# One level of Strassen's scheme for the x w_a and x w_b products of two gated layers, in tiles of 768 tokens

## The reference, cut to what matters

```python
def _attn_ref(q, k, v, g_norm):            # q, k, v: 4 batches, 8 heads, 576 tokens, 64
    kv = np.einsum('bhsd,bhse->bhde', k, v)
    out = np.einsum('bhsd,bhde->bhse', q, kv)
    rms = np.sqrt(np.mean(out * out, axis=-1, keepdims=True) + 1e-06)
    return (out / rms * g_norm).astype(np.float32)

def _moe_ref(x, w_a, w_b, w_out):          # x: 2304 x 512, w_a, w_b: 512 x 1536, w_out: 1536 x 512
    return (((x @ w_a) * (x @ w_b)) @ w_out).astype(np.float32)

def _moe2_ref(x, w_gate, w_val, w_out):
    gate = 1.0 / (1.0 + np.exp(-(x @ w_gate)))
    return ((gate * (x @ w_val)) @ w_out).astype(np.float32)
```

## Time and profile before

| | us |
|---|---|
| runs shown: median (lowest to highest, 3 runs) | 1001.93 (998.65 to 1002.4) |
| profiled execution: span from first to last instruction | 998.2 |
| median less span | 3.7 |
| attention, up to the first matmul of a layer | 93.3 |
| the two layers, to the last matmul | 901.5 |
| TensorE busy | 978.8 (98%) |
| DVE busy / ACT busy / POOL busy | 508.2 / 444.2 / 16.7 |

### The profile page before, as it was taken

One profiled execution on the slowest core, in us unless ns is written; L12 is line 12 of the kernel. 1 busy time (PEld: TensorE's weight loads), 2 busy tenths in 40 slices (PEclk: granted clock), 3 DMA queues, 4 the chain that ended last, 5 costly groups with the idle time before them and its releaser, 6 DMA issues.

```text
span 998.2 us, 14895 instructions
## 1 busy us (share of the span) xinstructions
PE 978.8 (98%) x5744; PEld 945.2 (95%) x5744; DVE 508.2 (51%) x742; ACT 444.2 (45%) x755; POOL 16.7 (2%) x84
## 2 busy tenths in 40 slices
PE   7799999999999999999999999999999999999998
PEld 7688999999999999999999999999999999999997
DVE  1357545545545545545545545545545545545543
ACT  2368434434434434434434434434434435434433
POOL 1112000000000000000000000000000000000000
PEclk8899999999999999999999999999999999999999
DMA  9995200000000000000543000000000000000000
GB/s 230 241 245 158 78 1 0 0 0 0 0 0 0 0 0 0 0 0 1 150 126 105 1 1 32 0 0 32 0 0 32 0 0 31 0 0 27 6 1 32
DMA packets 41132, 38.15 MB, mean 38 GB/s; under 512 B 1936, under 2 KB 35728, under 8 KB 41104
## 3 DMA queue, kind: packets, MB, share of 16 engines
q1 hardware_dynamic: 41104, 37.76, 14.5%
HBM read 33.03 MB, written 4.72 MB: 38 GB/s over the span
## 4 chain that ended last, share of the span: by engine, by line
PE 93%; DMA 2%; SPq 2%; ACT 1%; DVE 0%; issue 0%; POOL 0%; POOLq 0%
PE bank L372 60%; PE bank L419 15%; PE bank L421 15%; DMA qkv_even<-in_v_dram 2%; SPq L215 2%; PE bank L330 1%; PE bank L344 1%; PE bank L355 1%; ACT x L466 1%; PE bank L318 0%; ACT squares L452 0%; DVE normed L563 0%; ACT qT L442 0%; SPq L239 0%; DVE kv L538 0%
## 5 line engine op out<-in xcount | busy, mean ns | idle before, releaser
L372 PE MATMUL bank<-x_hi,ab_hi 128*128 128x384 f32 x1152 | 385.7, 335 | 0.0
L372 PE MATMUL bank<-x_hi,ab_lo 128*128 128x384 f32 x1152 | 385.7, 335 | 0.0
L372 PE MATMUL bank<-x_lo,ab_hi 128*128 128x384 f32 x1152 | 385.3, 334 | 0.0
L585 DVE TENSOR_TENSOR wo_lo<-w_raw,wo_hi 128x512 fp32r<-128x512 f32 x144 | 99.5, 691 | 236.1 <-ACT wo_hi L485 236.1
L372 PEld LDWEIGHTS bank<-x_hi,ab_hi 128*128 128x128 f32 x1152 | 216.3, 188 | 2.9
L372 PEld LDWEIGHTS bank<-x_lo,ab_hi 128*128 128x128 f32 x1152 | 216.3, 188 | 2.8
L372 PEld LDWEIGHTS bank<-x_hi,ab_lo 128*128 128x128 f32 x1152 | 216.2, 188 | 0.0
L572 DVE TENSOR_TENSOR ab_lo<-w_raw,ab_hi 128x1024 fp32r<-128x1024 f32 x144 | 176.3, 1225 | 53.2 <-ACT ab_hi L471 52.1
L488 ACT ACTIVATE h_hi<-qkv_even 128x384 fp32r<-128x384 f32 x144 | 75.8, 526 | 248.3 <-DVE qkv_even L589 248.3
L482 ACT ACTIVATE qkv_even<-bank 128x384 f32<-128x384 f32 x144 | 70.9, 492 | 254.4 <-PE bank L372 254.2
L471 ACT ACTIVATE ab_hi<-w_raw 128x1024 fp32r<-128x1024 f32 x144 | 150.4, 1044 | 0.0
(11 more groups left out here) (49 smaller groups left out, 533.0 us busy)
## 6 DMA issues: line engine op xcount, KB each, us to landing
w_raw<-in_moe_w_out_dram SPq DMA_DIRECT2D x24, 256.0 KB, 4.4
out_dram<-qkv_even SPq DMA_DIRECT2D x18, 256.0 KB, 2.0
w_raw<-in_moe_w_a_dram SPq DMA_DIRECT2D x12, 256.0 KB, 5.3
w_raw<-in_moe_w_b_dram SPq DMA_DIRECT2D x12, 256.0 KB, 5.6
w_raw<-in_moe_w_gate_dram SPq DMA_DIRECT2D x12, 256.0 KB, 3.0
w_raw<-in_moe_w_val_dram SPq DMA_DIRECT2D x12, 256.0 KB, 3.4
w_raw<-in_q_dram SPq DMA_DIRECT2D x2, 1152.0 KB, 17.1
qkv_even<-in_k_dram SPq DMA_DIRECT2D x4, 288.0 KB, 5.3
```

The lines of the kernel that those rows point to most:

```text
L372: last = pe.matmul(acc[:, 0:TILE], w[:, m % 2, at], xx[:, c, :], start=(c == 0 and n_pass == 0), stop=(c == KC - 1 and n_pass == 2))
L585: dve.tensor_tensor(wo_lo[:, m % 2, :], w_raw[:, m, 2 * HALF:3 * HALF], wo_hi[:, m % 2, :].bitcast(F32), ALU.subtract).then_inc(wo_lo_read ...
```

## The change

The hidden products of both layers are computed by Winograd's form of Strassen's scheme. The unit is 512 features by 256 hidden features (one of w_a or w_b, so 12 units in a tile) by 768 tokens. Cut in two along each side it is eight block products; the scheme makes seven, each of 6 matmuls of 384 columns (2 chunks of features times 3 passes). It needs four sums of weight blocks per unit and four sums of token blocks per tile (both on POOL, into `s_raw` and `t_raw`), and seven sums or copies of the block products per unit: in `bank[0]` to `bank[3]` three products are added to what four others left there. All seven weight blocks (14 x 128 columns per unit) and all seven token blocks (5376 columns per tile) are split into hi and lo.

The tile grows from 384 to 768 tokens, 3 per layer. TensorE runs `project` of an earlier hidden chunk in pairs of matmuls between the products of a unit. A tile has 24 project steps (12 chunks, 2 halves of 384 tokens): 10 beside units 2 to 11, and 14 behind them. The first half's accumulators are drained after step 11 (the engines reach it in their order behind the splits of step 13), the second's at the end; in that stretch the tokens of the next tile are split too. Weights are no longer kept: SP loads 512 KB per unit and 256 KB per project step, each a few steps ahead. The hardware loops are gone; every tile is written out. The splits for the first tile move to attention steps 17 to 24. In layer 1 the sigmoid of three of the four blocks is one ACT instruction of 1152 elements per pair of units. `out_sb` takes the place of `h1`.

In the diff below the POOL, SP, TensorE and DVE orders are shown. ACT's has the same form as DVE's: in a unit `s1` (copy of product 1), `split_h` in even units, in layer 1 the sigmoid in odd units, `split_w` group 0, `s5` (copy of product 3), group 1, `split_wo`, `a11` (copy or sigmoid of product 5's bank) in even units, group 2, `split_h` in odd ones; then the same last stretch. `split_w` has three groups: 512, 1024 (the sums from POOL) and 256 columns. `split_x` is 768 columns.

```diff
+    HT = 384
+    TT = 2 * HT
+    TILES = TOKENS // TT
+    PAIRS = CHUNKS // 2
+    UNITS = 2 * PAIRS
+    STEPS_OF_TILE = 2 * CHUNKS
...
-    SPLIT_W_AT = {13: 0, ALL_STEPS: 1}
-    EARLY_CHUNKS = len(SPLIT_W_AT)
-    SPLIT_X_AT = {9: (0,), 10: (1,), 11: (2,), 12: (3,)}
+    W_PREP_AT = 17
+    X_PREP_AT = {18: (0,), 19: (1,), 20: (2,), 21: (3,), 22: (4,), 23: (5,), 24: (6,)}
+    POOL_W_AT, POOL_T_AT = 13, {16: (0,), 17: (1,), 18: (2,), 21: (3,)}
...
+            def load_unit(u):
+                if u >= 2:
+                    sp.wait_ge(w_lo_ready, 3 * (u - 2) + 3)
+                sp.dma_start(w_raw[:, u % 2, :, :],
+                             layer_weights[layer][which][:, j * 2 * P:(j + 1) * 2 * P].rearrange("(c p) f -> p c f", p=P)
+                             ).then_inc(w_loaded[u % 2], 16)
...
+            def sum_weights(u):
+                pool.wait_ge(w_loaded[z], 16 * (u // 2 + 1))
+                if u >= 1:
+                    pool.wait_ge(w_lo_ready, 3 * (u - 1) + 2)
+                pool.tensor_tensor(s_raw[:, 1, :, :], a21_, a22_, ALU.add).then_inc(s_raw_ready, 1)
+                pool.tensor_tensor(s_raw[:, 2, :, :], a11_, a21_, ALU.subtract).then_inc(s_raw_ready, 1)
+                pool.wait_ge(s_raw_ready, 4 * u + 1)
+                pool.tensor_tensor(s_raw[:, 0, :, :], s_raw[:, 1, :, :], a11_, ALU.subtract).then_inc(s_raw_ready, 1)
+                pool.wait_ge(s_raw_ready, 4 * u + 3)
+                pool.tensor_tensor(s_raw[:, 3, :, :], a12_, s_raw[:, 0, :, :], ALU.subtract).then_inc(s_raw_ready, 1)
...
+            def sum_tokens(tau, i):
+                in0, in1 = ((b12, b11), (b22, t[0]), (b22, b12), (b21, t[1]))[i]
+                pool.tensor_tensor(t[i], in0, in1, ALU.subtract).then_inc(t_raw_ready, 1)
...
+            def last_block(u):
+                g = u // 2
+                pool.wait_ge(u3_ready, u + 1)
+                pool.wait_ge(s5_ready, u + 1)
+                if g >= 1:
+                    pool.wait_ge(h2_ready, 2 * g)
+                pool.tensor_tensor(c_sb[:, u % 2, 2, :], u3[:, :], s5[:, :], ALU.add).then_inc(c22_ready, 1)
...
+            for tau in range(ALL_TILES):
+                for v in range(UNITS):
+                    if unit(tau, v) + 1 < ALL_UNITS:
+                        sum_weights(unit(tau, v) + 1)
+                    last_block(unit(tau, v))
+                    if tau + 1 < ALL_TILES and v in (5, 7, 9):
+                        sum_tokens(tau + 1, (v - 5) // 2)
+                if tau + 1 < ALL_TILES:
+                    sum_tokens(tau + 1, 3)
...
+            def product(tau, v, i):
+                u = unit(tau, v)
+                if v == 0:
+                    pe.wait_ge(x_lo_ready, 7 * tau + i + 1)
+                if i == 0:
+                    pe.wait_ge(w_lo_ready, 3 * u + 1)
+                    if u:
+                        pe.wait_ge(u2_ready, u)
+                elif i == 1:
+                    pe.wait_ge(w_lo_ready, 3 * u + 2)
+                    if u and v % 2:
+                        pe.wait_ge(a11_ready, u // 2 + 1)
+                    elif u:
+                        pe.wait_ge(h1_ready, 2 * (u // 2 - 1) + 1)
+                elif i == 2 and u:
+                    pe.wait_ge(c12_ready, u)
+                elif i == 3 and u:
+                    pe.wait_ge(c21_ready, u)
+                elif i == 4:
+                    pe.wait_ge(s1_ready, u + 1)
+                elif i == 5:
+                    pe.wait_ge(s5_ready, u + 1)
+                elif i == 6:
+                    pe.wait_ge(u3_ready, u + 1)
+                    pe.wait_ge(w_lo_ready, 3 * u + 3)
+                to, at = product_bank(u, ROLE[i]), W_PLACE[i]
+                for c in range(2):
+                    for n_pass, (w, xx) in enumerate(((w_hi, x_hi), (w_hi, x_lo), (w_lo, x_hi))):
+                        last = pe.matmul(to[:, 0:HT], w[:, u % 2, at, c, :], xx[:, i, c, :],
+                                         start=(OPENS[i] and c == 0 and n_pass == 0),
+                                         stop=(c == 1 and n_pass == 2), skip_group_check=True)
+                last.then_inc(product_done, 1)
...
+                        if m == 0 and n_pass == 0:
+                            if n == 0:
+                                pe.wait_ge(x_ready, ALL_STEPS)
+                            elif a in ACT_ACCS[(2 * tau + half - 1) // (2 * TILES)]:
+                                pe.wait_ge(act_drained, act_before(tau, half) - 2 + (0, 0, 1)[a] + 1)
+                            else:
+                                pe.wait_ge(dve_drained, dve_before(tau, half))
...
+            for tau in range(ALL_TILES):
+                for v in range(UNITS):
+                    behind = project(tau, v - 2) if v >= 2 else iter(())
+                    for i in range(7):
+                        if tau or v or i >= 2:
+                            product(tau, v, i)
+                        if i:
+                            for _ in range(2):
+                                next(behind, None)
+                    for _ in behind:
+                        pass
+                for q in range(CHUNKS - 2, STEPS_OF_TILE):
+                    for _ in project(tau, q):
+                        pass
...
+            for tau in range(ALL_TILES):
+                layer = tau // TILES
+                for v in range(UNITS):
+                    u, w, j = unit(tau, v), v % 2, v // 2
+                    g = pair(tau, j)
+                    dve.wait_ge(product_done, 7 * u + 2)
+                    dve.wait_ge(s1_ready, u + 1)
+                    if u:
+                        dve.wait_ge(c21_ready, u)
+                    dve.tensor_tensor(u2[:, :], product_bank(u, 1)[:, 0:HT], s1[:, :], ALU.add).then_inc(u2_ready, 1)
+                    if w == 0 and v:
+                        split_h(tau, v - 1)
+                    split_w(u + 1, 0)
+                    dve.wait_ge(product_done, 7 * u + 4)
+                    dve.wait_ge(u2_ready, u + 1)
+                    if u:
+                        dve.wait_ge(c22_ready, u)
+                    dve.tensor_tensor(u3[:, :], product_bank(u, 3)[:, 0:HT], u2[:, :], ALU.add).then_inc(u3_ready, 1)
+                    split_w(u + 1, 1)
+                    if w == 1:
+                        to = h1_place(tau, j, 0)
+                        dve.wait_ge(product_done, 7 * u + 5)
+                        dve.wait_ge(a11_ready, g + 1)
+                        dve.tensor_tensor(to, product_bank(u, 0)[:, 0:HT], a11[:, :], ALU.mult).then_inc(h1_ready, 1)
+                    if v:
+                        split_wo(tau, v - 1)
+                    dve.wait_ge(product_done, 7 * u + 6)
+                    if g:
+                        dve.wait_ge(h2_ready, 2 * g - 1)
+                    dve.tensor_tensor(c_sb[:, w, 0, :], product_bank(u, 2)[:, 0:HT], u2[:, :], ALU.add).then_inc(c12_ready, 1)
+                    split_w(u + 1, 2)
+                    dve.wait_ge(product_done, 7 * u + 7)
+                    if g:
+                        dve.wait_ge(h1_ready, 2 * g)
+                    dve.tensor_tensor(c_sb[:, w, 1, :], product_bank(u, 3)[:, 0:HT], u2[:, :], ALU.add).then_inc(c21_ready, 1)
+                    if w == 1:
+                        if layer == 1:
+                            dve.wait_ge(gates_ready, g - pair(TILES, 0) + 1)
+                        dve.wait_ge(c12_ready, u + 1)
+                        dve.wait_ge(c21_ready, u + 1)
+                        to = h1_place(tau, j, 1)
+                        dve.tensor_tensor(to, c_sb[:, 1, 1, :], c_sb[:, 0, 1, :], ALU.mult).then_inc(h1_ready, 1)
+                        split_h(tau, v - 1)
+                        to = h2_place(tau, j, 0)
+                        dve.tensor_tensor(to, c_sb[:, 1, 0, :], c_sb[:, 0, 0, :], ALU.mult).then_inc(h2_ready, 1)
+                        to = h2_place(tau, j, 1)
+                        dve.wait_ge(c22_ready, u + 1)
+                        dve.tensor_tensor(to, c_sb[:, 1, 2, :], c_sb[:, 0, 2, :], ALU.mult).then_inc(h2_ready, 1)
+                dve.wait_ge(h1_ready, 2 * pair(tau, PAIRS))
+                dve.wait_ge(h2_ready, 2 * pair(tau, PAIRS))
+                split_h(tau, CHUNKS - 1)
+                split_wo(tau, CHUNKS - 1)
+                for q in range(CHUNKS, STEPS_OF_TILE):
+                    split_h(tau, q)
+                    split_wo(tau, q)
+                    if q == CHUNKS + 1:
+                        drain(tau, 0)
+                    if tau + 1 < ALL_TILES and q - CHUNKS < 7:
+                        split_x(tau + 1, q - CHUNKS)
+                drain(tau, 1)
```

More of the change, by code:

```diff
@@ L193, in done_before, with unit @@
-        def done_before(layer, t):
-            return count_before(layer, t, ACCS)
-        def columns(start, size):
-            return slice(start, start + size) if isinstance(start, int) else bass.ds(start, size)
-        def tile_of_x(c, t):
-            return x[:, c, columns(t * TILE, TILE)]
```

(24 more changed lines are left out.)

523 lines of the change are left out of this document (319 added, 204 removed).

## The result

The changed kernel takes 1014.26 us (median of 4, 1011.8 to 1015.05) where the kernel before takes 1002.16 on the same chip (998.65 to 1002.41): a ratio of 1.0131, 95% interval 1.0104 to 1.0158. It is 1.3% slower. The forecast was 963, with 938 to 997 as its range; the result lies above that and on the side that had a chance of 0.13, though not by the mechanism that stood there. The profiled execution's span is 1012.9 us, 14.7 above that of before.

A forecast was written before the change was run, and what follows sets the result against it. The layers were taken as bound by TensorE's matmul count alone. 998.2 - 74.9 (matmuls) + 6 (attention) + 17.3 (behind unit 11, drains) + 1.8 (unit 2) + 11 (POOL) = 959.4; with 3.7 for the median, 963 us, range 938 to 997.

The forecast's parts named there:

- the side that had a chance of 0.13: Outcome slower than the kernel before by more than half a per cent, 5 us; chance 0.13.
- What they cost DVE beside them: Cost to DVE of POOL's sums running beside it in the units: between nothing and 51 us, taken as 11 us.
- the middle price: 0.58 us for a POOL sum of 256 columns, between 0.31 for one pass and 0.84 for three.
- the bound of 51: Upper limit: h1 and h split each wait for one whole POOL sum of 0.84 us; 51 us.
- rival (a): Full exclusion: each chain operation waits out a whole POOL sum of 0.58 us; 32 us for 11, 984 us; chance 0.17.
- the estimate beside it: POOL's 256-column sum at about 0.6 us, from the skill page's 4497 ns for 2048 columns.
- the split of h at 10.4: In odd units DVE starts splitting h at 10.4 us, after c21 and the second h1 product; h_lo ready about 11.0.
- matmuls removed: Hidden matmuls fall from 3456 to 3024; the 432 that go, at 173.4 ns, save 74.9 us.
- attention, splits alone: Token and weight splits in attention's last steps add 6 us; 3 if TensorE covers half, 10 if POOL delays normalisation.
- behind unit 11 and the drains: TensorE waits 1.7 us for h_lo, then 1.4 (layer 0) or 0.95 us (layer 1) for drains; 17.3 us in six tiles.
- Rival (c): DVE and POOL never overlap and bound every unit at 11.0 us; 1093 us in all; chance 0.13.
- The clock: TensorE's clock stays at 1.00; waits of 1.7 us might bring it down, which wasn't expected.

The follow-up runs named there:

- e2_fill: Changed kernel with POOL's weight, token and last-block sums left out and fills that read nothing in their place; 964.4 us, once, span 962.6.
- e5_late_fill: Changed kernel with projections one unit later and POOL's sums replaced by fills; 943.96 us, once, span 942.2.
- e1_late: Changed kernel with each projection one unit later in TensorE's order, nothing else changed; 963.49 us, ratio 0.9623 to the kernel before.
- e4_late_tail: e1_late with the first half's drain ahead of step 13's splits and the seventh token split moved from step 18 to 21; 966.74 us, ratio 0.9642.
- e7_tail_only: Changed kernel with only the early drain and the seventh token split at step 21, without the late projection; 1017.76 us, once.
- e8_pool_tail: e4_late_tail with POOL's fourth token sum waiting for the tile's last w_out split, and the seventh token split behind step 23; 952.74 us, ratio 0.951.

## Why the prediction was wrong

**The step that failed** is "What they cost DVE beside them": between "nothing" and 51 us I took the middle price, half of it, twice: 11 us. The runs give 50.3 (changed kernel less e2_fill, one profiled execution of each). The mechanism was named; its price was the error. That 50.3 lies beside the bound of 51 is partly chance, since it is made up otherwise: 29 in units 4 to 10, 8 in unit 2 (9.5 less 1.4), 8.6 in the tail and 0.7 at the drains, nothing behind unit 11, 4 in attention (first product 5.7 earlier in e2_fill, unit 0 1.4 longer), less 1.5 for slow matmuls, of which e2_fill has more; 49 in all. Three things in my step were wrong.

First, "on average half of it" takes POOL and DVE for engines that meet by chance. They don't: all of POOL's idle time in a unit stands ahead of L370 and ends with DVE's `u` (340.7 us over 72 units, in the rows above). From there POOL runs through, last block, token sum, four weight sums, so it lies at the same place of every unit, and in odd ones that is where the chain stands. A whole sum per link, as in rival (a), is nearer to it.

Second, the price of a sum. An undisturbed sum of 256 columns takes 0.72 us (in attention, at 75.9), not 0.58 nor the 0.6 of the estimate beside it, and the token sums, 1.8 us undisturbed and 2.3 in the units, weren't on the chain at all in my sum; they are what makes waits of 0.7 us into waits of 1.6 to 1.8. Rival (a) named them ("later still behind token sums") and didn't price them.

Third, the places. Behind unit 11, where I had 3.5 us, POOL costs nothing: its weight sums stand behind the fourth token sum, and that waits for a token split. It starts in the tail instead, over steps 13 to 20, a place that I didn't have: 8.6 us. In layer 0 the cost there is not that DVE waits for POOL but that POOL's token sum waits for DVE.

Behind all three stands a choice that the prediction took over unseen: "the split of h at 10.4" is DVE's order. By data it could be made some 4 us earlier (312.5 for 316.55 in the unit above), and then neither POOL's sums nor the 1.7 us behind unit 11 need be on TensorE's path. That this is so is argued from the timeline, not run.

The rest of the sum, against the 959.4 forecast for a span of 1012.9. Since POOL's row is the difference to e2_fill, the rows below it are e2_fill's:

| step | forecast | measured | from |
|---|---|---|---|
| matmuls removed | -74.9 | -74.9 | 5312 of them at 0.1735 and 0.2315 us, e2_fill's units 9.36 to 9.55 |
| POOL beside DVE | 11 | 50.3 | span of the changed kernel less e2_fill |
| attention, splits alone | 6 | 8.2 | first product at 101.5 in e2_fill, 93.3 before |
| unit 0 | 0 | 5.1 | 12.37 us in e2_fill, for 7.28; 2.2 of it low clock |
| unit 2 | 1.8 | 1.4 | e2_fill |
| behind unit 11 and the drains | 17.3 | 15.1 | 11.4 + 3.7 in e2_fill |
| low clock in layer 1 | 0 | 4.6 | 24 matmuls in e2_fill, 0.14 to 0.2 us each |
| not accounted for | 0 | 4.9 | 1012.9 - 998.2 less the rows above |

Point by point. **Right**: the count of matmuls and their 173.4 ns; that unrolled code costs nothing; that SP's loads hide; that DVE alone holds a unit (e5_late_fill's units are TensorE-bound); the wait behind unit 11, 1.7 forecast and 1.67 to 1.68 measured in layer 0; the wait at step 12 in layer 0, 1.4 forecast, 1.24 measured.

**Layer 1** comes out otherwise. The wait behind unit 11 is 2.13 us for 1.7, in e2_fill too, so POOL isn't its cause. The prediction let product 7 end at 8.84 in both layers. That holds in layer 0, where two matmuls of projection stand behind it; in layer 1 the nine of a step are used up before it, and its last matmul ends the unit, at about 9.19. That is 0.35 us; another 0.1 lies between c21 and the h product (0.65 us from start to start in layer 0 of e2_fill, 0.76 in layer 1). The wait for the drains is 0.71 us in tile 3 for 0.95, and there is none in tiles 4 and 5: eight slow matmuls stand before it there and take longer than the wait would have been.

**Rival (c)**, DVE and POOL as the bound of every unit, is false in its strong form: odd units take 9.36 to 9.54 us also in the changed kernel, and e1_late keeps to that throughout with the same blocked operations. DVE works 83% of layer 0 there (308.9 of 372 us). It was the length of the chain, not the sum of the work.

**Unit 0** was put at 7.28 although its first two products stand between the transposes of the last attention steps. They could not be back to back. That was to be seen in the diff (`if tau or v or i >= 2`), not in the rows.

**The clock** was forecast to stay at its upper level. In unit 0, where TensorE had been waiting for attention's chain, it is at 0.50 for 10 matmuls, 1.8 of the 3.7 us that the unit is too long. And it falls behind the 2.13 us waits of layer 1. TensorE of the changed kernel behind unit 11 of tile 4:

```profile
828.59 0.47 PE L518 MATMUL bank<-wo_hi,h_hi 128*128 128x512 f32 x1 [1.97 <-DVE h_lo L772]
...
829.60 0.60 PE L518 MATMUL bank<-wo_lo,h_hi 128*128 128x512 f32 x1
830.00 0.63 PE L518 MATMUL bank<-wo_hi,h_lo 128*128 128x512 f32 x1
```

Eight matmuls of 512 columns follow at 0.4 to 0.43 us (granted clock 0.50 from 829.9 to 832.9, so 1.2 GHz), then the pace is 0.23 again and the clock 1.00. It is the same in tile 5, not in tile 3, whose wait was as long; in e2_fill it is in all three. The waits of 1.6 to 1.8 us in the units show nothing of the sort.

**What stays open**: the 4.9 us in distances too small to name (some tiles of the runs have units of 9.54 us in place of 9.36 with no wait in them); what DVE's h split is worth in an earlier place; why the fourth token sum is held in layer 0 and not in layer 1; and attention. Its first product came at 107.2, 108.9, 108.0, 109.6 and 110.8 us in five kernels with the same code there (the changed one, e1_late, e4_late_tail, e7_tail_only, e8_pool_tail), each profiled once, so its terms are good to some 3 us only.

## What to carry to other kernels

Where one engine waits for another's result, ask first what that result needs by data and what merely stands ahead of it in the other engine's order. Then give it a whole stage of slack: one changed offset in the order of `project` was worth 50 us, 5%, and made the blocking of DVE harmless without removing any of it. Work that is put on POOL because POOL is idle still takes SBUF time from DVE, or waits for DVE; add its durations to DVE's wherever DVE's operations have two SBUF inputs, and put it where DVE has nothing due. And when two engines release each other, don't price their meeting at an average: here it came at the same place of unit after unit.

## What the runs showed of the hardware

- POOL sums of 256, 384 and 768 columns with two SBUF inputs took 0.72 to 0.74, 1.01 and 1.8 us undisturbed, the one of 384 beside DVE's 1024-column split 1.93; a copy of 256 columns 0.39, a fill 0.31. Only the fill left DVE's 684 ns as it was.
- The blocked operation can be tiny: 96x8 numbers, 0.16 us alone and 1.77 behind a POOL sum.
- DVE operations with one input out of PSUM kept their 548 to 557 ns beside POOL in every run.
- POOL can be held far longer than by one operation of DVE: a 768-column sum that starts while DVE has ten splits with two SBUF inputs ahead took 8.5 us for 1.8 in all three tiles of layer 0, a copy in its place 7.5. In layer 1, and in layer 0 with the order of e4_late_tail, the sum took 2.1, and DVE was held.
- A TensorE wait of 2.13 us within a stream otherwise full was followed by seven to nine slow matmuls at a granted clock of 0.50 in 11 of 15 places (five kernels), 1.5 us more; waits of up to 1.8 us in the same kernels were not.
